# A fused FFT mixer and feed-forward kernel: the pair stage reordered around a min/relu threshold, other orders between stages, weights split by three engines

## What is computed

```python
X = np.fft.rfft(x, axis=1)                  # x: (4, 3008, 256)
Yr = Xr @ w_r - Xi @ w_i + b_r              # 256 x 256 weights
Yi = Xr @ w_i + Xi @ w_r + b_i
Y  = sign(Y) * max(|Y| - 0.01, 0)           # each part by itself: the threshold, lam = 0.01
y = np.fft.irfft(Y, n=3008, axis=1)
h = y.reshape(12032, 256) @ w_in            # 256 x 2048
g = max(h, 0) + alpha * min(h, 0)
out = g @ w_out                             # 2048 x 256
```

## Time and profile before

| | us |
|---|---|
| median of 3 runs | 1493.46 (1493.42 to 1493.47) |
| profiled execution, its own time | 1494.51 |
| span of that execution | 1492.7 |
| busy: TensorE | 1414.5 (95%) |
| busy: VectorE | 958.1 (64%) |
| busy: ScalarE | 692.2 (46%) |
| busy: GpSimd | 282.3 (19%) |

### The profile page before, as it was taken

How to read it: one execution, slowest core, us unless ns; L and a number is a source line. 1 busy time by engine, 2 the same in 40 slices (tenths; PEclk the granted TensorE clock), 3 DMA queues, 4 the chain that set the end, 5 groups by cost and what they waited for, 6 DMA issues and landing times.

```text
span 1492.7 us, 21894 instructions
## 1 busy us (share of the span) xinstructions
PE 1414.5 (95%) x7184; PEld 1191.1 (80%) x7184; DVE 958.1 (64%) x1887; ACT 692.2 (46%) x1580; POOL 282.3 (19%) x281
## 2 busy tenths in 40 slices
PE   7885699999999999999999999999999999999997
PEld 3783478888888778888888877888888888888886
DVE  6695447787775545777776555777776555555554
ACT  3452335555554444554554444555554444444442
POOL 1341532122110142122110033121120100011000
PEclk9996899999999999999999999999999999999999
DMA  7453222213111043132221043222211111011100
GB/s 240 128 153 121 86 88 58 64 49 80 49 45 39 24 128 98 45 76 57 69 54 27 20 108 96 53 62 67 64 45 29 31 30 25 1 30 30 20 14 14
DMA packets 162765, 93.93 MB, mean 63 GB/s; under 512 B 110941, under 2 KB 140253, under 8 KB 162653
## 3 DMA queue, kind: packets, MB, share of 16 engines
q1 hardware_dynamic: 162652, 92.54, 23.3%
HBM read 55.00 MB, written 37.49 MB: 62 GB/s over the span
## 4 chain that ended last, share of the span: by engine, by line
PE 80%; DVE 9%; issue 3%; ACT 3%; POOL 2%; DMA 2%; SPq 1%; ACTq 0%; DVEq 0%
PE out_ps L365 32%; PE h_ps L365 31%; PE work_ps L365 11%; PE work_ps L451 2%; POOL x_lo L850 2%; DVE g_raw L752 1%; ACT negpart L596 1%; DVE g_lo L687 1%; PE work_ps L399 1%; PE work_ps L452 1%; DMA turned<-in_moe_w_out_dram 1%; DVE turned L779 1%; DVE x_hi L693 1%; DVE clamped L723 1%; DVE shrunk L728 1%
## 5 line engine op out<-in xcount | busy, mean ns | idle before, releaser
L752 DVE SCALAR_TENSOR_TENSOR g_raw<-negpart,keep,h_ps 128x502 f32<-128x502 f32 (+1 forms) x384 | 282.8, 737 | 399.4 <-ACT negpart L596 397.1
L596 ACT ACTIVATE negpart<-h_ps 128x502 f32<-128x502 f32 (+1 forms) x384 | 226.1, 589 | 501.6 <-PE h_ps L365 499.3
L365 PE MATMUL out_ps<-g_hi,wout_hi 128*128 128x502 f32 (+1 forms) x768 | 311.4, 406 | 5.1 <-DVE g_lo L687 3.1
L365 PE MATMUL h_ps<-y_lo,win_hi 128*128 128x502 f32 (+1 forms) x768 | 301.2, 392 | 0.0
L365 PE MATMUL h_ps<-y_hi,win_hi 128*128 128x502 f32 (+1 forms) x768 | 300.0, 391 | 1.2 <-DVE y_lo L743 1.2
L365 PE MATMUL out_ps<-g_hi,wout_lo 128*128 128x502 f32 (+1 forms) x768 | 298.4, 388 | 0.0
L365 PE MATMUL out_ps<-g_lo,wout_hi 128*128 128x502 f32 (+1 forms) x768 | 298.3, 388 | 0.0
L365 PE MATMUL h_ps<-y_hi,win_lo 128*128 128x502 f32 (+1 forms) x768 | 298.0, 388 | 0.0
L687 DVE TENSOR_TENSOR g_lo<-g_raw,g_hi 128x502 fp32r<-128x502 f32 (+1 forms) x384 | 270.6, 705 | 0.1
L605 ACT ACTIVATE g_hi<-g_raw 128x502 fp32r<-128x502 f32 (+1 forms) x384 | 236.1, 615 | 0.7 <-DVE g_raw L752 0.3
L365 PEld LDWEIGHTS out_ps<-g_hi,wout_hi 128*128 128x128 f32 x768 | 145.7, 190 | 33.8 <-issue 6.5
(11 more groups left out here) (78 smaller groups left out, 1904.8 us busy)
## 6 DMA issues: line engine op xcount, KB each, us to landing
fwd_scratch<-staging SPq DMA_DIRECT2D x64, 192.0 KB, 2.1
table<-in_twiddles_dram SPq DMA_DIRECT2D x32, 384.0 KB, 3.7
pair_raw<-fwd_scratch SPq DMA_DIRECT2D x96, 128.0 KB, 2.1
inv_scratch<-inv_sb SPq DMA_DIRECT2D x96, 128.0 KB, 1.7
back_raw<-inv_scratch SPq DMA_DIRECT2D x64, 192.0 KB, 2.7
x_raw<-in_x_dram SPq DMA_DIRECT2D x64, 160.0 KB
out_dram<-turned SPq DMA_DIRECT2D x128, 40.0 KB, 2.0
out_dram<-turned SPq DMA_DIRECT2D x64, 48.0 KB, 1.8
```

The source lines that it names most:

```text
L365: mm = pe.matmul(ps, lhs, rhs, start=(first and n == 0), stop=(last and n == len(terms) - 1), **kw)
L596: act.activation(negpart[:, q % 2, 0:size], h_ps[:, q % 2, 0:size], ACT.Relu, scale=-1.0).then_inc(negpart_done, 1)
L752: dve.scalar_tensor_tensor(g_raw[:, q % 2, 0:size], negpart[:, q % 2, 0:size], keep[:, m:m + 1], h_ps[:, q % 2, 0:size], ALU.mult, ALU.add ...
```

## The change

- The threshold is computed as min(v + lam, relu(v - lam)). VectorE adds the bias (`add_bias`), ScalarE computes above = relu(biased - lam) (`find_above`, with a bias tile `low` of -lam), VectorE computes shrunk = min(biased + lam, above) in one `scalar_tensor_tensor` (`shrink`). `clamped` and its instruction are gone.
- In the pair loop of group 0 VectorE's order is add_bias, rest_spec, shrink, rest_pair, rest_shrunk. In the tiles add_bias stays one step after forward2, at the end of the step; shrink, split_shrunk and rest_shrunk come two steps after it. TensorE's order in the tiles is unchanged.
- The forward stage has 16 units (S_MID is gone), the late one 5 (S_LATE), whose loads are issued in the pair loop, and the first two of which are split in it. The 11 other forward units of group 1 are placed in tile 0 and at the start of tile 1. Stores and back loads of the late stage have another order, and the first six inverse units have six PSUM banks instead of two.
- Weight chunks 0 and 1 are loaded at the start of the pair loop and split by VectorE alone in it; 2 and 3 are loaded in it. In tile 0 SP loads chunk m/2 + 4 at each even step; ScalarE makes both hi parts, VectorE win_lo, GpSimd wout_lo, with a semaphore for each lo part.
- The last tile's twelve stores are issued by SP and ScalarE, six each.

The diff, without semaphore lists and most unchanged lines:

```diff
@@ -45,8 +45,8 @@
-S_MID, S_LATE = 3, 6
-S_EARLY = S_HEAD + S_MID + S_LATE
+S_LATE = 5
+S_EARLY = S_HEAD + S_LATE
@@ -57,8 +57,9 @@
-    s = max(S_HEAD * (f // 6 + 1), S_EARLY) + f % 6 * STEPS + m - 1
-    return s if f < TILES - 6 and f % 6 * STEPS + m >= 1 and s < S_HEAD * (f // 6 + 2) else None
+    at = f % 6 * STEPS + m - 1
+    s = S_HEAD * (f // 6 + 1) + at
+    return s if f < TILES - 6 and 0 <= at < S_HEAD and s >= S_EARLY else None
@@ -187,7 +189,9 @@
         def i_bank(u):
-            return work_ps[:, 2 + u % 2 if u < I_HEAD else 3, 0:4 * NA]
+            if 2 <= u < 4:
+                return out_ps[:, u - 2, 0:4 * NA]
+            return work_ps[:, (0, 1, None, None, 2, 3)[u] if u < I_HEAD else 3, 0:4 * NA]
@@ -268,29 +281,22 @@
-                    sp.wait_ge(w_lo_done, w - 1)
+                    sp.wait_ge(win_lo_done, w - 1)
+                    sp.wait_ge(wout_lo_done, w - 1)
...
-            for s in range(S_HEAD + S_MID):
-                load_x(s + X_RING)
+            for s in range(S_HEAD):
+                if s + X_RING < S_HEAD:
+                    load_x(s + X_RING)
@@ -302,10 +308,13 @@
-                if s in (10, 12):
-                    load_table(s // 2 - 5)
+                if s == 10:
+                    load_table(0)
...
+            load_table(1)
+            load_ffw(0)
+            load_ffw(1)
@@ -313,28 +322,36 @@
-                if k in (13, 16):
-                    load_ffw(k // 3 - 4)
+                if k in (5, 7, 9, 11):
+                    load_x(S_HEAD + (k - 5) // 2)
+                if k in (12, 15):
+                    load_ffw(k // 3 - 2)
+                if k == PAIRS - 1:
+                    load_x(S_HEAD + X_RING)
...
-            for n in range(S_LATE):
-                s = S_HEAD + S_MID + n
+            store_fwd(S_HEAD)
+            store_fwd(S_HEAD + 1)
+            load_back(0)
+            load_back(1)
+            store_fwd(S_HEAD + 2)
+            load_back(2)
+            for s in range(S_HEAD + 3, S_EARLY):
+                store_fwd(s)
+            for s in range(S_HEAD + 1, S_EARLY):
...
-                store_fwd(s)
-                if n in (1, 2, 4):
-                    load_back(n // 2)
...
+                    if f == 0 and m % 2 == 0:
+                        load_ffw(m // 2 + 4)
...
-                        store_out(f - 1, 2 * (m - 4))
-                        store_out(f - 1, 2 * (m - 4) + 1)
+                        store_out(sp, f - 1, 2 * (m - 4))
+                        store_out(sp, f - 1, 2 * (m - 4) + 1)
...
-                    if f == 0 and m % 2 == 0:
-                        load_ffw(m // 2 + 2)
@@ -350,8 +367,8 @@
-            for n in range(12):
-                store_out(TILES - 1, n)
+            for n in range(0, 12, 2):
+                store_out(sp, TILES - 1, n)
@@ -438,12 +455,14 @@
-                if u < 2:
+                if u >= I_HEAD:
+                    pe.wait_ge(y_lo_done, u)
+                elif u < 2:
+                    pe.wait_ge(inv_copied, PAIRS)
+                elif u < 4:
+                    pe.wait_ge(biased_done, PAIRS)
+                else:
...
-                elif u < I_HEAD:
-                    pe.wait_ge(y_lo_done, u - 1)
-                else:
-                    pe.wait_ge(y_lo_done, u)
@@ -459,7 +478,7 @@
-                    pe.wait_ge(w_lo_done, m // 2 + 1)
+                    pe.wait_ge(win_lo_done, m // 2 + 1)
@@ -477,7 +496,9 @@
-                    pe.wait_ge(biased_done, PAIRS)
+                    pe.wait_ge(y_lo_done, I_HEAD)
+                if f == 0 and m % 2 == 0:
+                    pe.wait_ge(wout_lo_done, m // 2 + 1)
@@ -563,6 +584,12 @@
+            def find_above(p):
+                act.wait_ge(biased_done, p + 1)
+                if p >= 1:
+                    act.wait_ge(shrunk_done, p)
+                act.activation(above[:, :], biased[:, p % 2, :], ACT.Relu, bias=low[:, :]).then_inc(above_done, 1)
+
@@ -604,14 +631,16 @@
-            def split_win(w):
+            def split_ffw(w):
...
+                act.activation(wout_hi[:, w, :, :].rearrange("p m e -> p (m e)"), ffw_raw(w)[:, 2 * DIM:4 * DIM],
+                               ACT.Copy).then_inc(wout_hi_done, 1)
...
-            for s in range(S_HEAD + S_MID):
+            for s in range(S_HEAD):
@@ -620,32 +649,38 @@
-                if s == 15:
-                    split_tw(0)
-                    split_itw(0)
+            split_tw(0)
+            split_itw(0)
...
+            act.wait_ge(low_ready, 1)
...
+                    find_above(k - 1)
+                if 2 <= k + 3 < PAIRS:
+                    split_pair(k + 3)
+                if 0 <= k - 1 < PAIRS:
...
-                if 2 <= k + 3 < PAIRS:
-                    split_pair(k + 3)
...
-            split_win(0)
...
-                copy_fwd(S_HEAD + S_MID + n)
-                if n in (3, 4, 5):
-                    split_back(n - 3)
-            split_win(1)
-            for u in range(I_HEAD):
+                copy_fwd(S_HEAD + n)
+                if n == S_LATE - 2:
+                    split_back(0)
+            split_back(1)
+            split_y(0)
+            split_y(1)
+            split_back(2)
+            for u in range(2, I_HEAD):
...
+            act.wait_ge(win_hi_done, 2)
+            act.wait_ge(wout_hi_done, 2)
@@ -671,15 +706,20 @@
                     if f == 0 and m % 2 == 0 and m // 2 + 2 < CHUNKS:
-                        split_win(m // 2 + 2)
+                        split_ffw(m // 2 + 2)
                     p = p_unit(f, m, -4)
...
                         split_itw(p // 3)
+                    p = p_unit(f, m, 2)
+                    if p is not None:
+                        split_shrunk(p)
                     p = p_unit(f, m, 1)
                     if p is not None:
-                        split_shrunk(p)
+                        find_above(p)
             split_bent(TILES - 1, STEPS - 1)
+            for n in range(1, 12, 2):
+                store_out(act, TILES - 1, n)
@@ -712,21 +752,20 @@
-            def shrink(p):
+            def add_bias(p):
                 dve.wait_ge(mix_mm, p + 1)
...
                 dve.tensor_tensor(biased[:, p % 2, :], mix_bank(p), bias[:, :], ALU.add).then_inc(biased_done, 1)
-                dve.wait_ge(biased_done, p + 1)
-                if p >= 1:
-                    dve.wait_ge(shrunk_done, p)
-                dve.tensor_scalar(clamped[:, :], biased[:, p % 2, :], LAM, -LAM, ALU.min, ALU.max).then_inc(clamped_done, 1)
-                dve.wait_ge(clamped_done, p + 1)
+
+            def shrink(p):
+
+                dve.wait_ge(above_done, p + 1)
                 if p >= 2:
...
                     dve.wait_ge(shr_lo_done, p - 1)
-                dve.tensor_tensor(shrunk[:, p % 2, :], biased[:, p % 2, :], clamped[:, :],
-                                  ALU.subtract).then_inc(shrunk_done, 1)
+                dve.scalar_tensor_tensor(shrunk[:, p % 2, :], biased[:, p % 2, :], LAM, above[:, :], ALU.add,
+                                         ALU.min).then_inc(shrunk_done, 1)
@@ -758,10 +797,30 @@
-            def copy_wout(w):
-                dve.wait_ge(ffw_loaded[w % 2], 32 * (w // 2 + 1))
-                dve.tensor_copy(wout_hi[:, w, :, :].rearrange("p m e -> p (m e)"),
-                                ffw_raw(w)[:, 2 * DIM:4 * DIM]).then_inc(wout_hi_done, 1)
+            def split_ffw(w, step):
+                raw = ffw_raw(w)
+                if step == 0:
+                    dve.wait_ge(ffw_loaded[w % 2], 32 * (w // 2 + 1))
+                    dve.tensor_copy(win_hi[:, w, :, :].rearrange("p h f -> p (h f)"),
+                                    raw[:, 0:2 * DIM]).then_inc(win_hi_done, 1)
+                if step == 1:
+                    dve.tensor_copy(wout_hi[:, w, :, :].rearrange("p m e -> p (m e)"),
+                                    raw[:, 2 * DIM:4 * DIM]).then_inc(wout_hi_done, 1)
+                if step == 2:
+                    rest_win(w)
+                if step == 3:
+                    dve.wait_ge(wout_hi_done, w + 1)
+                    rest(wout_lo[:, w, :, :].rearrange("p m e -> p (m e)"), raw[:, 2 * DIM:4 * DIM],
+                         wout_hi[:, w, :, :].rearrange("p m e -> p (m e)")).then_inc(wout_lo_done, 1)
+
+            def rest_win(w):
+                dve.wait_ge(win_hi_done, w + 1)
+                rest(win_lo[:, w, :, :].rearrange("p h f -> p (h f)"), ffw_raw(w)[:, 0:2 * DIM],
+                     win_hi[:, w, :, :].rearrange("p h f -> p (h f)")).then_inc(win_lo_done, 1)
+
+            def rest_back(v):
+                dve.wait_ge(back_hi_done, v + 1)
+                rest(back_lo[:, v % 2, :], back_raw[:, v % 2, :], back_hi[:, v % 2, :]).then_inc(back_lo_done, 1)
@@ -781,7 +840,8 @@
-            for s in range(S_HEAD + S_MID):
+            dve.memset(low[:, :], -LAM).then_inc(low_ready, 1)
+            for s in range(S_HEAD):
@@ -792,22 +852,27 @@
-                    shrink(k - 1)
+                    add_bias(k - 1)
...
```

(67 more changed lines are left out.)

12 lines of the change are left out of this document (6 added, 6 removed).

## The result

The changed kernel takes 1566.4 us (median; 1563.2 to 1567.2 in four runs) against 1493.5 before: a ratio of 1.048, with a 95% interval of 1.046 to 1.050. It is slower by 72.9 us. The forecast was 1539, with 1505 to 1568 for its range: the direction is right, and the time lies 1.6 us inside the upper end, nearer to rival (c)'s 1562 than to the forecast.

The account below looks back on a forecast made before the run. TensorE bounds from 215.1 us on, busy 1249.7 of 1264.9 us; slack lies before. 1494.5 - 4.3 - 5 - 14.5 - 16.5 - 2.8 + 88.8 = 1540.2, or 1539 in terms of the median; range 1505 to 1568.

Parts of the forecast that it names:

- rival (c): Whole kernel: waits come, but loads hold the first stages, so only 20 of 43 us gained; 1562 us, chance 0.09.
- The pairs inside the tiles: Tiles with pairs: late shrinkage makes TensorE wait at inverse2 in 72 pairs, plus 88.8 us, bounds 60 to 110.
- The rule on VectorE and GpSimd: VectorE instructions with two SBUF inputs or in two-port mode and GpSimd instructions reading SBUF exclude each other throughout.
- rival (d): Tiles with pairs: waits also drop TensorE's clock to 0.87, 78 us more, 1617 us; chance 0.03.
- The first tile: First tile: earlier weight loads and splits end ScalarE's load waits, minus 16.5 us, bounds 11 to 20.
- From the last pair to the first tile: Last inverse2 before the tiles to first hidden product: reordered loads, stores and units, minus 14.5 us, bounds 11 to 18.
- Pair stage: Pair loop before the tiles: clamp moved to ScalarE as relu and reordering, minus 5 us, bounds 2 to 9.
- Forward stage: Start to first forward2: pair loads go out without S_MID's stores ahead, minus 4.3 us, bounds 3 to 6.4.
- Last stores: Kernel's end: twelve store issues split over two queues, minus 2.8 us, bounds 2 to 3.
- (a): Pairs in the tiles: no wait at inverse2, early gains stand alone; 1450 us, chance 0.09.
- (b): Pairs in the tiles: wait is short, about 0.4 us per pair, +29; 1479 us, chance 0.05.
- remark on the minimum: VectorE's new min has both inputs in SBUF, so it stays exposed to GpSimd's exclusion as the clamp was.

Follow-up runs that it names:

- The two experiments that move either end of the chain: Changed kernel with inverse2, its copy and store one step later in the tiles: 1468.2 us; changed kernel with the shrinkage back at step one: 1466.2 us.
- the one that makes the kernel before late: Kernel before the change with only shrink, split_shrunk and rest_shrunk two steps after forward2 instead of one: 1664.6 us, ratio 1.115.
- the kernel with the minimum earlier: Changed kernel, shrinkage still two steps late, but VectorE computes the minimum ahead of the spectrum rest and rest_shrunk right behind that rest: 1504.3 us.
- the weights' edit: Changed kernel with SP's load_ffw at the end of tile 0's even steps instead of the head: 1561.4 us; on the shrinkage-at-step-one kernel 1466.6, repeated 1465.0.

## Why the prediction was right, and where its sizes were off

**The pairs inside the tiles** decided, as forecast, and by the mechanism forecast. The waits, by the starts of 72 inverse2, sum to 87.0 us against 88.8, within 2%. Of 24 in a group nine wait 1.03 to 1.10 (forecast: ten at 1.1), five 1.23 to 1.31 (seven at 1.3 to 1.4), five 0.26 to 0.82 (six at 0.4 to 0.8) and five 1.8 to 2.64 (one at 2.6, four others lengthened by 0.6 to 2). The two experiments that move either end of the chain remove it, and the one that makes the kernel before late brings it back. The rule on VectorE and GpSimd that the prediction leaned on shows again in the step above: 1.21 and 1.22 us for subtractions that take 0.42 alone.

**The size of that term was too small by 12.5 us**, 101.3 instead of 88.8. A wait costs more than its length. First, after a wait inverse2's second matmul starts 0.22 us behind the first in the median, where it was 0.12 before: 6.2 us over the 72. Second, the granted clock falls seven times to 0.50, that is to 1.2 GHz, for a short stretch, each time within 1.5 us behind 1.69 to 2.48 us of idle time at inverse2 (fifteen waits have 1.65 or more). In these stretches 75 matmuls start at about twice their usual distance, 9.9 us together. One of the stretches, and the clock over a longer piece around it (us, busy time, clock):

```profile
607.50:610.90 3.40, 3.40 (x12) 2.88 (x12) 0.42 (x1) 0.51 (x1) 0.00 (x0) 0.50 0.11 39
...
600.00:660.00 60.00, 52.13 (x272) 44.06 (x271) 34.88 (x71) 27.77 (x68) 9.21 (x11) 0.94 0.17 47
```

Against this, the waits for spec_lo, 4.2 us in this stage before, are down to 0.8, since mixing now comes later. 87.0 + 6.2 + 9.9 - 3.4 = 99.7, which leaves 1.6 us of the 101.3. The same account fits the kernel with the minimum earlier: 35 + 6.2 + 1.5 (one such stretch) - 3.4 = 39 us, where its twelve tiles are 39.9 longer than before. The prediction had the lower clock only in its upper bound and as rival (d); it came in small pieces, about an eighth of that rival's 78 us.

**The first tile gave 8.5 instead of 16.5.** The failed step is "behind it stand load_back and the stores of x units, which have two steps of room": load_back has none, and moving the weights behind it gives back 3.8 us here. The step also allowed nothing for TensorE's waits for GpSimd's x_lo in this tile, 3.3 us in six waits. That the second is worth its full length is argued from the 3.0 and 4.1 us by which the first tile was shorter with x_lo on VectorE. By the starts, against the distance that each kind of matmul has in the later tiles, TensorE loses 11.3 us in this tile where 5.3 were forecast: 6.0 of the 8.0 missing. It lost 23.2 before, not 24.6, and the added work is 3.4, not 2.8, which is the rest. With the weights last and x_lo on VectorE the loss is 5.6.

**From the last pair to the first tile 12.0 instead of 14.5.** The forecast had 14.9 us for this stretch, and it took 17.4. Half of the 2.5 us is the start: the first reading back is issued 4.4 us after the last inverse2, at 113.15, and not 3.2 after it, and the third follows 1.3 late, at 117.60. The other half is its landing: the term took the median, 2.7, and it was split at 121.61, beside stores and loads of x. In the six other profiles without the weights' edit, where it takes 2.5 to 3.1, the same stretch is 14.8 to 16.7 us.

**Pair stage 3.8 instead of 5.** Up to the last but one inverse2 it is 5.0 us shorter, with steps of 2.4 to 2.6 us for the most part, as forecast. The missing 1.2 is the last inverse2 (VectorE and TensorE, changed kernel):

```profile
105.35 0.42 DVE L733 CAST x_hi<-x_raw 94x512 fp32r<-94x512 f32 x1
...
105.81 0.69 DVE L727 TENSOR_TENSOR x_lo<-x_raw,x_hi 94x512 fp32r<-94x512 f32 x1
106.42 0.41 DVE L759 TENSOR_TENSOR biased<-out_ps,bias 128x256 f32<-128x256 f32 x1
...
108.79 0.38 PE L382 MATMUL work_ps<-shr_hi,itw_hi 128*128 128x256 f32 x1 [2.69 <-DVE shr_lo L727]
```

Its wait was 1.50 before. The input split for the next forward unit, moved into the loop, now stands ahead of the last pair's bias: 0.42 + 0.69 = 1.1 us. The prediction counted what that split saves after the loop, and not what it holds up within. The other split that was moved costs as much two steps earlier, where inverse2 follows inverse2 after 3.35 us instead of 2.15, and is contained in the 5.0.

**Smaller terms.** Forward stage 5.4 instead of 4.3: the first pair load is issued at 35.41, not at 36.1, and the first forward2 follows it after 3.1 us instead of 3.5. Last stores 1.7 instead of 2.8: the twelve issues take 3.1 us on two queues instead of 5.83 on one, as forecast, but the last one lands 2.3 us after its issue has ended, where it was 1.3 before. The prediction had left this landing unchanged. The other tiles grew by 2.1 us, 1.8 of it in tiles 18 to 22, which have no pair, at equal instruction counts; this was not explained.

In all the profiled execution came out 26.2 us above the forecast's sum: 12.5 in the pairs, 2.1 in the other tiles, 11.6 in the gains around them. Every term but the forward stage's was off to the same side, so little of the range was left. Rival (c), which is nearer in the number, is not what happened: it had 20 of the 43 us of early gains, and 31.5 came. Rivals (a) and (b) fall with the waits, 1.2 us in the mean.

The prediction's remark on the minimum holds in part: beside GpSimd it takes 1.5 us in three places of the changed kernel, and with the shrinkage at step one up to 2.34, yet its mean in the pair stage is 0.45, where the clamp had 0.625.

## What to carry to other kernels

When work is moved to a later step, look where its consumer stands, not how busy its engine is: VectorE was busy 58% of the time here, and one step of delay cost 100 us, since the in-order TensorE stood in front of the one matmul that wanted the result. Place a chain's start and its consumer as a pair, and leave a whole step between them if a buffer allows it: in the kernel with inverse2 one step later VectorE's longer subtractions, 1.2 instead of 0.4 us, cost no wait. When you price a wait, add what follows it. And test a bundle of edits part by part: this one, without the late step, was a gain of 27 us.

## What the runs showed of the hardware

- After a wait of TensorE at inverse2 the second matmul starts 0.22 instead of 0.12 us behind the first, in the median of 72. Behind seven of the fifteen longest waits, 1.65 to 2.49 us of idle time, a short stretch at a granted clock of 0.50 followed and cost some 1.4 us each, though the clock of the whole stage reads 0.99. Together that is 16 us over 72 waits.
- ScalarE's relu with a bias takes 0.51 us for 128x256, a rounding copy of the same shape 0.42.
- A subtraction of 94x512 takes 0.69 us on VectorE and 1.28 on GpSimd, and while GpSimd runs one, VectorE's take up to four times as long: a win_lo of 128x512, 0.69 alone, took 2.59 beside a back_lo of 1.29 and a wout_lo of 1.26, one behind the other.
- A reading back of 192 KB issued beside stores and loads lands after 2.5 to 3.1 us in seven profiles and after 3.8 to 4.5 in four, at nearly the same program ahead of it.
